# Second MLP of a fused attention and two-MLP kernel: every chunk of the second product in float32r parts, and one eighth of the high parts written by VectorE instead of ScalarE

## What is computed

```python
attn = mab(x, mab(inducing, x))                  # (2, 12480, 128)
y = moe(attn.reshape(24960, 128), w_in, w_out, a, b)   # first MLP, a rational function between its products
# second MLP:
h = y @ w2_in                                    # (24960, 2048)
g = h * np.cos(h)
out = g @ w2_out                                 # (24960, 128)
```

## Time and the profile before

| | |
|---|---|
| median of three runs | 2633.49 us (2632.07 to 2635.88) |
| the profiled execution | 2632.91 us, span in the trace 2631.1 us |
| PE busy over the span | 2584.3 us (98%) |
| ACT busy | 2423.3 us (92%) |
| DVE busy | 2341.6 us (89%) |
| POOL busy | 2052.3 us (78%) |
| PE clock granted, mean over the span | 0.989 of full speed |

### The profile page before, as it was taken

How to read it: one execution, slowest core, us unless ns; L and a number is a source line. 1 busy time by engine, 2 the same in 40 slices (tenths; PEclk the granted TensorE clock), 3 DMA queues, 4 the chain that set the end, 5 groups by cost and what they waited for, 6 DMA issues and landing times.

```text
span 2631.1 us, 38615 instructions
## 1 busy us (share of the span) xinstructions
PE 2584.3 (98%) x10691; PEld 1794.6 (68%) x10691; DVE 2341.6 (89%) x2730; ACT 2423.3 (92%) x3173; POOL 2052.3 (78%) x1474
## 2 busy tenths in 40 slices
PE   8699999999999999999999999999999999999999
PEld 5366656665666666665656688888888888888887
DVE  4599999999999999999999888888888888888887
ACT  5499999999999999999999899999999999999998
POOL 0189999999999999999999777777777777777776
PEclk9699999999999999999999999999999999999999
DMA  7000000000002000000000000000000000000000
GB/s 220 21 8 11 10 8 11 7 11 7 11 17 71 8 11 7 11 8 11 7 11 5 1 12 12 12 11 11 11 11 11 11 11 11 11 11 11 11 11 15
DMA packets 25688, 45.52 MB, mean 17 GB/s; under 512 B 2888, under 2 KB 11880, under 8 KB 25384
## 3 DMA queue, kind: packets, MB, share of 16 engines
q1 hardware_dynamic: 25640, 44.92, 5.7%
HBM read 16.99 MB, written 12.78 MB: 11 GB/s over the span
## 4 chain that ended last, share of the span: by engine, by line
PE 62%; POOL 14%; issue 10%; DVE 8%; ACT 4%; DMA 1%; POOLq 1%; DVEq 0%; ACTq 0%; SPq 0%
PE bank L1166 22%; PE bank L1158 20%; POOL work L379 8%; PE bank L1016 8%; PE bank L1023 8%; DVE work L776 5%; POOL work L367 3%; POOL part_hi L389 2%; ACT work L532 2%; DVE bank L758 1%; PE bank L947 1%; PE bank L1149 1%; ACT work L520 1%; POOL part_hi L383 1%; DVE work L767 1%
## 5 line engine op out<-in xcount | busy, mean ns | idle before, releaser
L446 POOL TENSOR_TENSOR act_lo<-work,act_hi 128x960 fp32r<-128x960 f32 (+1 forms) x416 | 723.4, 1744 | 330.1 <-ACT act_hi L607 322.1
L1023 PE MATMUL bank<-work,v 128*128 128x480 f32 x1664 | 742.5, 568 | 0.2 <-ACT tokens_t L539 0.2
L1016 PE MATMUL bank<-part_hi,stack_now 96*128 96x480 f32 x2496 | 665.0, 400 | 13.7 <-DVE stack_next L704 7.1
L379 POOL TENSOR_TENSOR work<-work 128x960 f32<-128x960 f32 x278 | 621.9, 2237 | 42.3 <-POOL work L367 3.4
L912 DVE SCALAR_TENSOR_TENSOR work<-work,bank 128x960 f32<-128x960 int32 x416 | 479.6, 1153 | 155.3 <-ACT work L594 155.3
L1016 PEld LDWEIGHTS bank<-part_hi,stack_now 96*128 96x128 f32 x2496 | 434.9, 189 | 241.8 <-DVE work L776 161.9
L758 DVE SCALAR_TENSOR_TENSOR bank<-bank,over_c,work 128x960 f32<-128x960 f32 x416 | 508.4, 1222 | 42.8 <-PE bank L1016 34.1
L776 DVE SCALAR_TENSOR_TENSOR work<-bank,coef_a,work 128x960 f32<-128x960 f32 x416 | 502.2, 1207 | 0.2 <-PE bank L1016 0.2
L515 ACT ACTIVATE work<-work,made 128x960 f32<-128x960 f32 x416 | 469.1, 1128 | 26.2 <-POOL work L379 26.2
L594 ACT ACTIVATE work<-bank 128x960 int32<-128x960 f32 x416 | 404.2, 972 | 93.1 <-PE bank L1158 93.1
L918 DVE TENSOR_TENSOR work<-work,bank 128x960 f32<-128x960 f32 x416 | 477.2, 1147 | 0.0
(11 more groups left out here) (120 smaller groups left out, 3039.3 us busy)
## 6 DMA issues: line engine op xcount, KB each, us to landing
x_group<-tokens_t SPq DMA_DIRECT2D x52, 240.0 KB, 2.2
out_dram<-work SPq DMA_DIRECT2D x52, 240.0 KB, 2.4
x_ring<-in_x_dram SPq DMA_DIRECT2D x40, 240.0 KB, 6.1
work<-in_x_dram SPq DMA_DIRECT2D x12, 240.0 KB, 4.0
stack_now<-stack_next SPq DMA_DIRECT2D x8, 288.0 KB, 3.0
work<-in_moe_w_in_dram SPq DMA_DIRECT2D x1, 1024.0 KB, 15.4
w_raw<-in_moe_w_in_dram SPq DMA_DIRECT2D x1, 1024.0 KB, 4.9
v<-in_moe_w_out_dram SPq DMA_DIRECT2D x2, 0.5 KB, 13.9
```

Source lines behind the costliest of these rows:

```text
L379: nc.gpsimd.tensor_tensor(quot[k % 3], square[k % 3], abs_h[k % 3], ALU.add).then_inc(den_ready, 1)
L446: nc.gpsimd.tensor_tensor(act2_lo[:, k % 2, w], angle[k % ANGLES][:, w], act2_hi[:, k % 2, w].bitcast(F32), ALU.subtract).then_inc(act2_pa ...
L1016: mm = pe.matmul(place_out[:, t, :], stack_now[:, i, w], part_hi[0:K3, place, :], start=start, stop=stop, skip_group_check=not start)
L1023: mm = pe.matmul(sums, v[:, 2 * u + t, :], g[:, t * GROUP:(t + 1) * GROUP], start=(2 * u + t == 0), stop=(2 * u + t == CHUNKS - 1))
```

## The change

The second product is made of float32r parts for every unit and both halves, so the plain float32 matmul is gone and every unit has six matmuls there. For that, odd units need high and low parts of all 960 columns. Where k % 4 is 3 (`high_to`), ACT casts only the first half and DVE writes the high part of the second half itself, into a new buffer `hi_rest`, as the product of cosine and bank with a float32r output, ahead of L918 (now L934) which it then waits for. POOL makes the low part of such a unit in two halves, the second from `hi_rest`. `part_v2` splits all four chunks of each four.

```diff
+        hi_rest = at(work_at + 4 * (8 * UNIT + GROUP), "hi_rest", [P, GROUP], F32R)[:, :]
-        def split_to(k):
-            return GROUP if k % 2 else UNIT
+        def high_to(k):
+            return GROUP if k % 4 == 3 else UNIT
...
             def part_v2(j):
-                c = slice(4 * j, 4 * j + 3)
+                c = slice(4 * j, 4 * j + 4)
...
             def low_part(n0, k):
-                n, w = n0 + k, slice(0, split_to(k))
+                n = n0 + k
                 pool.wait_ge(act2_hi_ready, n + 1)
-                nc.gpsimd.tensor_tensor(act2_lo[:, k % 2, w], angle[k % ANGLES][:, w], act2_hi[:, k % 2, w].bitcast(F32),
-                                        ALU.subtract).then_inc(act2_parted, 1)
+                q, lo, hi = angle[k % ANGLES], act2_lo[:, k % 2, :], act2_hi[:, k % 2, :].bitcast(F32)
+                if high_to(k) == UNIT:
+                    nc.gpsimd.tensor_tensor(lo, q, hi, ALU.subtract).then_inc(act2_parted, 1)
+                else:
+                    nc.gpsimd.tensor_tensor(lo[:, 0:GROUP], q[:, 0:GROUP], hi[:, 0:GROUP], ALU.subtract).then_inc(act2_first_parted, 1)
+                    pool.wait_ge(act2_rest_ready, n0 // 4 + (k + 1) // 4)
+                    nc.gpsimd.tensor_tensor(lo[:, GROUP:], q[:, GROUP:], hi_rest.bitcast(F32), ALU.subtract).then_inc(act2_parted, 1)
...
                     q = halves(angle[j % ANGLES])
                     dve.wait_ge(cos_ready, n + 1)
+                    if high_to(j) < UNIT:
+
+                        if not isinstance(n, int) or n >= 4:
+                            dve.wait_ge(act2_used, n - 3)
+                        else:
+
+                            dve.wait_ge(act_used, UNITS)
+                        nc.vector.tensor_tensor(hi_rest, angle[j % ANGLES][:, GROUP:], buf(j)[:, 1, :], ALU.mult).then_inc(act2_rest_ready, 1)
+                        dve.wait_ge(act2_rest_ready, n0 // 4 + (j + 1) // 4)
                     nc.vector.tensor_tensor(q, q, buf(j), ALU.mult).then_inc(act2_ready, 1)
...
                 pe.wait_ge(act2_hi_ready, n + 1)
-                parted = split_to(k) // GROUP
+                his = [act2_hi[:, b, 0:GROUP], act2_hi[:, b, GROUP:]]
+                if high_to(k) < UNIT:
+                    pe.wait_ge(act2_rest_ready, n0 // 4 + (k + 1) // 4)
+                    his[1] = hi_rest
                 for t in range(2):
-                    if t < parted:
-                        mm(v2_hi, act2_hi[:, b, :], t, first=True)
-                        mm(v2_lo, act2_hi[:, b, :], t)
-                    else:
-                        mm(v2, angle[k % ANGLES], t)
+                    mm(v2_hi, his[t], t, first=True)
+                    mm(v2_lo, his[t], t)
                 pe.wait_ge(act2_parted, n + 1)
-                for t in range(parted):
-                    end = mm(v2_hi, act2_lo[:, b, :], t, last=(t == parted - 1))
+                for t in range(2):
+                    end = mm(v2_hi, act2_lo[:, b, t * GROUP:(t + 1) * GROUP], t, last=(t == 1))
```

More of the change, by code:

```diff
@@ L274, in bass_set_attention_two_mlps @@
         hid2_ready, turns_ready, angle_ready, cos_ready = (sem(n) for n in ("hid2_ready", "turns_ready", "angle_ready", "cos_ready"))
-        act2_ready, act2_hi_ready, act2_parted, act2_used = (sem(n) for n in ("act2_ready", "act2_hi_ready", "act2_parted", "act2_used"))
+        act2_ready, act2_hi_ready, act2_rest_ready, act2_first_parted, act2_parted, act2_used = (
+            sem(n) for n in ("act2_ready", "act2_hi_ready", "act2_rest_ready", "act2_first_parted", "act2_parted", "act2_used"))
         y_hi_ready, y_parted, out_t_ready = sem("y_hi_ready"), sem("y_parted"), sem("out_t_ready")
         out_turned, out_ready, out_written = sem("out_turned"), sem("out_ready"), sem("out_written")
-        def split_to(k):
-            return GROUP if k % 2 else UNIT
+        def high_to(k):
+            return GROUP if k % 4 == 3 else UNIT
         def y_place(g):
@@ L599, in unit2 @@
                 if k + HIGH >= 0 and exists_unit(n0 + (k + HIGH)):
-                    n, j, w = n0 + (k + HIGH), k + HIGH, slice(0, split_to(k + HIGH))
+                    n, j, w = n0 + (k + HIGH), k + HIGH, slice(0, high_to(k + HIGH))
                     act_.wait_ge(act2_ready, n + 1)
@@ L1165, in mm @@
                     c = 2 * u + t
-                    return pe.matmul(sums, lhs[:, c, :], rhs[:, t * GROUP:(t + 1) * GROUP], start=(c == 0 and first),
+                    return pe.matmul(sums, lhs[:, c, :], rhs, start=(c == 0 and first),
                                      stop=(u == GROUP_UNITS - 1 and last))
                 pe.wait_ge(act2_hi_ready, n + 1)
-                parted = split_to(k) // GROUP
+                his = [act2_hi[:, b, 0:GROUP], act2_hi[:, b, GROUP:]]
+                if high_to(k) < UNIT:
+                    pe.wait_ge(act2_rest_ready, n0 // 4 + (k + 1) // 4)
+                    his[1] = hi_rest
                 for t in range(2):
-                    if t < parted:
-                        mm(v2_hi, act2_hi[:, b, :], t, first=True)
-                        mm(v2_lo, act2_hi[:, b, :], t)
-                    else:
-                        mm(v2, angle[k % ANGLES], t)
+                    mm(v2_hi, his[t], t, first=True)
+                    mm(v2_lo, his[t], t)
                 pe.wait_ge(act2_parted, n + 1)
-                for t in range(parted):
-                    end = mm(v2_hi, act2_lo[:, b, :], t, last=(t == parted - 1))
+                for t in range(2):
+                    end = mm(v2_hi, act2_lo[:, b, t * GROUP:(t + 1) * GROUP], t, last=(t == 1))
                 return end
```

## The result

The changed kernel takes 2635.77 us in the median of 12 runs (2633.09 to 2640.05), the kernel before 2631.86 us (12 runs). The medians lie 3.9 us (0.15%) apart. The ratio of the runs is 1.0018, with a 95% interval of 1.001 to 1.0025: 0.18% slower, just inside the 0.2% that counted as no change, though the interval reaches a little beyond it. The prediction was 2637 us, +3 us over the profiled execution of the kernel before.

What follows compares the result with a forecast made beforehand. TensorE's own work was taken as the bound. Waits of 0.68 us a group (35.4 us) and 1 us at the end against 33.3 saved gave +3 us on 2632.9; with 0.6 us for the median, 2637 us, range 2618 to 2652.

Steps and rivals of the forecast that it cites:

- TensorE's saving: Second product of odd units: 1.46 us becomes 1.30, 0.16 us saved in each of 208 units, 33.3 us in all.
- The case in which no wait comes: Rival: all engines stay below TensorE's new 21.2 us a group and nothing waits, 2600 us; chance 0.10.
- The half product: VectorE's new product of 480 columns into hi_rest, in steps 0 and 4 of each group: 0.65 us, bounds 0.57 and 1.15.
- The waits: TensorE per group: `begin2` late by 0.47 us in step 0 and 0.13 in step 4, GpSimd's low part 0.08.
- ScalarE's lag in step 4: Full casts make ScalarE's step 2.65 us against TensorE's 2.60; 0.10 us of step 4's 0.13 us wait.
- the two waits overlap: Step 0's 0.47 us wait moves back TensorE's need for the low part, leaving 0.08 of GpSimd's 0.55 us.
- The rival in which they add: Last rival: GpSimd's backlog adds to VectorE's wait, 0.47 + 0.13 + 0.55 = 1.15 us a group, 2660 us; chance 0.18.
- The start: Longer `part_v2` on GpSimd ahead of the first cast, where GpSimd has nothing else; 2.2 us if its cover is gone.
- The end: Last unit's low part takes 2 x 1.23 us instead of 1.23 with TensorE waiting: 1 us.
- the first rival: The waits don't come, groups of 21.2 us: 2600 us; chance 0.10.
- the second: Rival with half the waits: weights load ahead, ScalarE's lag does not build up, 0.35 us a group, 2617 us; chance 0.12.
- a lock: If `hi_rest`'s product held GpSimd off, 1.3 us a group would put GpSimd at 21.6 us, the bound.

Runs made afterwards that it cites:

- tensor_only: Changed kernel without VectorE's half product and the added low parts, odd units' second halves multiplied with first-half parts: 2598.77 us, ratio 0.9881 to the kernel before.
- reduce_behind: Changed kernel with VectorE's full product first and hi_rest made from it behind, by a reduction over a one-element axis: 2630.41 us, ratio 0.9997 to the kernel before.
- scalar_casts_all: Changed kernel with ScalarE casting the full high part for every unit and no half product on VectorE: 2631.67 us, ratio 1.0008 to the kernel before.
- low_y_later: Changed kernel with the low part of y on GpSimd two steps later than its high part: 2630.36 us, ratio 1.0004 to the kernel before.
- reduce_both: Changed kernel with hi_rest reduced from the full product behind it, and y's low part two steps later: 2611.48 us, ratio 0.9928 to the kernel before.
- copy_behind: Changed kernel with VectorE's full product first and hi_rest made behind it as a float32r copy of its second half: 2671.0 us, ratio 1.0161 to the kernel before.

## Why the prediction was right

**TensorE's saving.** Costed 0.64 us a group, 33.3 us. `tensor_only` gave 31 us (interval 27 to 35), 0.62 us a group by the mean group times. The distance of 216 ns from the rows held, against the 202.5 that the prediction worked out from the Trainium skill, "TensorE: Matmul & The Clock Gate", "Wait — 56ns, not 53.3ns?": by that estimate 42 us should have come out. The case in which no wait comes was put at 2600 us from a kernel before of 2633.5, and that kernel ran at 2598.8 beside one of 2630.3.

**The half product.** Taken as 0.65 us, the 104 of them take 648 ns in the mean. The following product starts 0.03 us behind its end, as in the earlier trace rows: 2022.09 + 0.66 and then 2022.78.

**The waits.** Costed 0.47 us in step 0, 0.13 in step 4 and 0.08 for the low part; read, in the mean of 49 groups, 0.49, 0.06 and 0.09. The sum is 0.65 against 0.68. The one term that was off is ScalarE's lag in step 4, put at 0.10 us. In step 0 the lag is there: L601 starts at 2019.99, 0.15 us behind the end of `begin2` (2019.46 + 0.38 = 2019.84), where it was 0.04. In step 4 it does not reach VectorE, because the copy L905 stands between and ends after L601:

```profile
2009.03 0.98 ACT L601 ACTIVATE work<-bank 128x960 int32<-128x960 f32 x1
2009.53 0.68 DVE L905 COPY work<-bank 120x512 f32<-120x512 f32 x1
2010.13 1.14 DVE L919 SCALAR_TENSOR_TENSOR work<-work,bank 128x960 f32<-128x960 int32 x1
```

L601 has ended at 2010.01, the copy ends at 2010.21, and L919 starts with the copy's end. Without the 0.10, step 4 costs 0.03 us by the prediction's sum, and 0.06 was read.

**That the two waits overlap** was the step on which the sum hung: 0.55 us for GpSimd alone, of which 0.08 should be left. `reduce_behind`, with the same work on GpSimd and no wait for VectorE, waits 0.60 us a group for the low part by start times. `scalar_casts_all`, `reduce_behind` and `low_y_later` each take one away and gain 2.6, 5.5 and 3.7 us over the changed kernel by their ratios; `reduce_both` takes both and gains 24. The rival in which they add (2660 us) is out. The reason given against it was that a delayed cast delays the start of the low part, not the time at which GpSimd is free. The trace fits that: behind the split of y, L450 starts at 2023.93 with the end of L437 (2022.75 + 1.21), while its cast had ended at 2021.76 + 1.01 = 2022.77.

**The start.** The longer `part_v2` was taken as covered. The first transposes of the second MLP start at 1526.7 us, and before at 1526.9, so it cost nothing.

**The end.** Costed 1 us. From the transposes in the last group's step 3 to the end of the span it was 2631.1 - 2618.45 = 12.7 us before and is 2635.3 - 2620.86 = 14.4 now, 1.8 us more. TensorE waits for three low parts in a row there (1.06, 0.64 and 0.76 us), not only for the last unit's. This term was mis-sized by 0.8 us.

**Small misses.** GpSimd's full low part takes 2.28 us now, not 2.26, which is 0.1 us a group that was not counted. Its idle time was to fall to about 100 us and fell to 82. The misses have both signs: about 1 us too much for the saving, 1.6 us too much for the waits, 0.8 us too little for the end. That the sum, +3 us, came so near to the 3.9 measured is in part the luck of their cancelling. The range of 2618 to 2652 us left out not only the first rival and half of the last but the second too (2617 us), so that more than 2 in 10 of the chances lay outside.

GpSimd was not held off by the product into `hi_rest`, as the prediction had it: L450 at 2.28 us is nowhere near the 0.65 us more that the prediction reckoned for a lock. `copy_behind` shows what such a lock looks like.

## What to carry to other kernels

When a wait disappears and the time stays, look for a second wait close behind it in the order. Here four different kernels, each without one of the two waits, lay within about 8 us of the kernel before, and only those without both gained (up to 26 us). Slack has to be computed per step of the order, from start times. All engines were below the bound in sum, and each of the two waits came from one bunch: 0.68 us in one step of VectorE, 1.83 us around one step of GpSimd. Spreading GpSimd's bunch over steps was worth more here than moving work to another engine.

## What the runs showed of the hardware that was not expected

A VectorE copy of 128 x 480 float32 to float32r from SBUF to SBUF took 0.41 to 2.05 us beside GpSimd instructions of 2.27 us (`copy_behind`). How long it took depended on when it began: in all 104 cases it ended 0.26 to 0.32 us behind the GpSimd instruction that was running. A reduction over an axis of one element, with the same source, target and values, took 0.65 us in all 104 cases (`reduce_behind`). With the copy this kernel took 43 us more than with the reduction, by their ratios.
